# Theta's tiles in three parts around the second attention's transposes and values, v ahead of q and k, and the sines of three tiles in a row

## What is computed

```python
# 1: masked attention over 8 heads of 64 channels (4 local, 4 strided)
attn = softmax(where(mask[h], 0.125 * q @ k.T, -1e9)) @ v         # x: (4, 576, 512)
# 2: mixing over tokens and channels
theta = x @ w_theta
y = w_tok_r @ (x * cos(theta)) + w_tok_i @ (x * sin(theta))
u = x + y
x2 = u + maximum(u @ w_ch, 0)
# 3: four causal attention experts, two of which count for each token
gate = softmax over the 2 largest of (x2 @ w_gate)
out = sum_e gate[e] * softmax(causal(0.125 * (x2 @ wq[e]) @ (x2 @ wk[e]).T)) @ (x2 @ wv[e]) @ wo[e]
```

## Times and profile before

| | us |
|---|---|
| median of 3 runs (630.7 to 634.88) | 632.44 |
| the profiled execution, whole | 630.41 |
| its span in the trace | 628.6 |
| PE busy | 561.1 (89%) |
| DVE busy | 355.3 (57%) |
| ACT busy | 260.8 (41%) |
| POOL busy | 125.1 (20%) |
| granted TensorE clock, mean | 0.973 of full |

### The profile page before, as it was taken

The page is one execution under the profiler, slowest core; times in us unless marked ns, Lnnn a source line. Parts: engine busy times, 40 slices in busy tenths (PEclk is TensorE's granted clock), DMA queues, the critical chain, the costliest instruction groups (busy, mean ns, idle before and its releaser), DMA issues.

```text
span 628.6 us, 11634 instructions
## 1 busy us (share of the span) xinstructions
PE 561.1 (89%) x4469; PEld 474.6 (75%) x4469; DVE 355.3 (57%) x835; ACT 260.8 (41%) x768; POOL 125.1 (20%) x128
## 2 busy tenths in 40 slices
PE   6776999999988989999988989999988889999777
PEld 4555679998865679998865679998856669998545
DVE  1466384666778641566778641575776832344462
ACT  1556263365442362365442362255533353112343
POOL 2012162001321142001321133001221215000110
PEclk9878999999999999999999989999989999999989
DMA  6900315321000012321000012330000010000002
GB/s 158 276 22 19 101 34 124 89 58 26 14 2 1 18 59 59 90 54 26 14 1 2 18 59 50 83 69 22 18 2 1 5 70 3 1 2 1 1 0 76
DMA packets 73413, 27.13 MB, mean 43 GB/s; under 512 B 68624, under 2 KB 68624, under 8 KB 73360
## 3 DMA queue, kind: packets, MB, share of 16 engines
q1 hardware_dynamic: 70992, 22.70, 14.5%
q10 hardware_dynamic: 2368, 3.70, 1.7%
HBM read 21.67 MB, written 4.72 MB: 42 GB/s over the span
## 4 chain that ended last, share of the span: by engine, by line
PE 72%; DVE 14%; ACT 6%; issue 4%; POOL 1%; ACTq 1%; DVEq 0%; POOLq 0%
PE acc L1126 34%; PE wide L1126 14%; PE wide L1210 4%; PE turned L1286 4%; PE wide L1189 3%; PE turned L1243 3%; PE turned L1230 3%; DVE xt L961 2%; PE turned L1152 2%; PE acc L1396 2%; ACT probs L757 2%; PE turned L1260 2%; PE wide L1174 1%; DVE probs L935 1%; DVE turns L983 1%
## 5 line engine op out<-in xcount | busy, mean ns | idle before, releaser
L689 POOL TENSOR_TENSOR probs<-probs,rec 96x768 f32<-96x768 f32 (+1 forms) x16 | 21.7, 1355 | 231.5 <-DVE rec L919 231.5
L764 ACT ACTIVATE probs<-wide,nmax 128x128 f32<-128x128 f32 (+4 forms) x72 | 39.1, 549 | 67.3 <-DVE nmax L904 64.9
L757 ACT ACTIVATE probs<-wide,nmax 96x128 f32<-96x128 f32 (+1 forms) x176 | 61.5, 370 | 10.3 <-issue 6.7
L772 ACT ACTIVATE pt<-turned 128x384 f32<-128x384 f32 (+3 forms) x64 | 30.9, 483 | 83.3 <-PE turned L1230 43.7
L698 POOL TENSOR_TENSOR probs<-probs,weight 128x128 f32<-128x128 f32 (+4 forms) x36 | 27.0, 769 | 167.4 <-DVE weight L942 167.4
L1126 PE MATMUL wide<-w_tok_hi,z_hi 128*128 128x288 f32 x216 | 46.8, 297 | 2.7 <-ACT o_sb L790 1.3
L948 DVE COPY pt<-turned 128x288 f32<-128x288 f32 (+4 forms) x72 | 32.0, 454 | 27.2 <-PE turned L1243 25.2
L1126 PE MATMUL wide<-w_tok_lo,z_hi 128*128 128x288 f32 x216 | 45.8, 293 | 0.0
L1126 PE MATMUL wide<-w_tok_hi,z_lo 128*128 128x288 f32 x216 | 45.8, 293 | 0.0
L711 POOL TENSOR_TENSOR z_lo<-absf,z_hi 128x512 fp32r<-128x512 f32 x20 | 28.3, 1415 | 70.2 <-ACT z_hi L820 70.2
L904 DVE TENSOR_REDUCE nmax<-wide 128x1 f32<-128x128 f32 (+4 forms) x72 | 32.7, 510 | 16.1 <-PE wide L1215 16.1
(11 more groups left out here) (170 smaller groups left out, 1491.2 us busy)
## 6 DMA issues: line engine op xcount, KB each, us to landing
raw_q<-in_q SPq DMA_DIRECT2D x32, 128.0 KB, 2.4
raw_k<-in_k SPq DMA_DIRECT2D x32, 128.0 KB, 2.4
out<-o_sb SPq DMA_DIRECT2D x16, 256.0 KB, 2.0
raw_v<-in_v SPq DMA_DIRECT2D x64, 31.5 KB
raw_v<-in_v SPq DMA_DIRECT2D x16, 120.0 KB
raw_r<-in_moe_w_tok_r ACTq DMA_DIRECT2D x1, 1152.0 KB, 9.0
stage<-in_moe_w_theta ACTq DMA_DIRECT2D x2, 512.0 KB, 5.5
raw_i<-in_moe_w_tok_i ACTq DMA_DIRECT2D x1, 1024.0 KB, 10.9
```

The source lines that it names most:

```text
L689: g.tensor_tensor(pr, pr, rec[0:rows, 1, 0:nt].unsqueeze(2).broadcast_to([rows, nt, w]), ALU.mult).then_inc(s["probs_pool"], 1)
L757: e = a.activation(probs[0:rows, hh, t * P:t * P + w], wide[slot][0:rows, t * P:t * P + w], ACT.Exp, bias=nmax[0:rows, hh, t:t + 1], accum ...
L764: e = a.activation(probs[:, hh, to0:to0 + n], wide[slot][:, at0:at0 + n], ACT.Exp, bias=nmax[:, hh, j:j + 1], accum_out=sums[:, hh, j:j + 1])
L772: ins = a.activation(dst, src, ACT.Copy)
```

## The change

It edits the lists of the bodies, and what a body's steps need for it:

- `theta` of tiles 0 to 3 becomes three steps on the contraction's four chunks: chunks 0 and 1 where the whole was (before turn 1), chunk 2 after turn 1, chunk 3 after the values. All three add into one place of `acc`, and the eviction stays at the slot's end. `slot_of_s3` no longer evicts at once between its steps.
- In the slots of stage 1 `v` comes ahead of `qk`: four v in slot 1; v 4, two qk and `rank` in slot 2; three qk in slot 3 and three in slot 4. Before: four qk; four v; v 4, `rank` and two qk; two qk. A slot's number is its place in FILL, from 0.
- `trig` 0, 1 and 2 stand together at the end of the slot with theta 3, ahead of `out` 0. `products` 0 goes ahead of the last unit's transposes, `products` 1 ahead of its values, and theta 4 is evicted ahead of `products` 1 (before: after the values).
- `last_slot` gives the order of the last unit's slot; in the epilogue it puts out 2, 3 and 4 behind the values (before, out 2 and 3 stood around turn 1).
- The first wave waits for its four PSUM places one by one, where it first writes each, rather than for all at its start.

```diff
@@ slot_of_s3
-    steps += gap[0] + [("turn",) + behind + (1,)]
-    if ahead:
-        steps += [("norm",) + ahead + (0,), ("exp",) + ahead + (1,)]
-    steps += at_once(gap[1]) + [("values",) + behind]
-    if ahead:
-        steps.append(("norm",) + ahead + (1,))
-    return steps + done(gap[0]) + at_once(gap[2]) + at_once(gap[3])
+    steps += gap[0] + [("turn",) + behind + (1,), ("norm",) + ahead + (0,), ("exp",) + ahead + (1,)]
+    steps += gap[1] + [("values",) + behind] + gap[2] + [("norm",) + ahead + (1,)]
+    return steps + done(gap[0] + gap[1] + gap[2]) + at_once(gap[3])
+def last_slot(behind, gap):
+    steps = gap[0] + [("turn",) + behind + (0,)] + gap[1] + [("turn",) + behind + (1,)] + gap[2]
+    return steps + [("values",) + behind] + gap[3]
...
+def theta_in_parts(m):
+    return [[("theta", m, 0, 2)], [("theta", m, 2, 3)], [("theta", m, 3, KC)]]
@@ FILL
-    [halves("qk", 0)[:1], halves("qk", 0)[1:], halves("qk", 2)[:1], halves("qk", 2)[1:]],
     [v_of(0), v_of(1), v_of(2), v_of(3)],
-    [v_of(4), [("rank",)], [("gexp",)] + halves("qk", 1)[:1], [("gate",)] + halves("qk", 1)[1:]],
-    [halves("qk", 3)[:1], halves("qk", 3)[1:]],
-    [theta(0)],
-    [theta(1)],
-    [theta(2)],
-    [theta(3), [], out_of(0)],
-    [theta(4), [("trig", 0), ("products", 0)] + out_of(1),
-     [("trig", 1), ("products", 1), ("split", 0)] + out_of(2, 3, 4)],
+    [v_of(4), halves("qk", 0)[:1], halves("qk", 0)[1:], [("rank",)]],
+    [halves("qk", 2)[:1], [("gexp",)] + halves("qk", 2)[1:], halves("qk", 1)[:1], [("gate",)]],
+    [halves("qk", 1)[1:], halves("qk", 3)[:1], halves("qk", 3)[1:]],
+    theta_in_parts(0),
+    theta_in_parts(1),
+    theta_in_parts(2),
+    theta_in_parts(3) + [[("trig", 0), ("trig", 1), ("trig", 2)] + out_of(0)],
+    [[("products", 0)], theta(4), at_once(out_of(1)) + [("done", "theta", 4), ("products", 1)],
+     [("split", 0)] + at_once(out_of(2, 3, 4))],
@@ FILL_LAST
-    [out_of(2), out_of(3), out_of(4)],
+    [[], [], [], at_once(out_of(2, 3, 4))],
@@ PE, wave
-                        for n in range(4):
-                            free(("wide", "acc")[n // 2], n)
...
+                            if m == 0 and n == 0:
+                                for i in ((0,), (1,), (2, 3))[o]:
+                                    free(("wide", "acc")[i // 2], i)
```

More of the change, by code:

```diff
@@ L61, with result @@
 EVICTED = ("channel", "qk", "v", "theta", "out")
+def result(step):
+    return step[:2] if step[0] == "theta" else step
 def done(steps):
-    return [("done",) + x for x in steps if x[0] in EVICTED]
+    return [("done",) + result(x) for x in steps if x[0] in EVICTED and x[3:] in ((), (KC,))]
 def at_once(steps):
@@ L86, in attention_steps @@
         if behind and behind[0] == "s3":
-            steps += slot_of_s3(ahead, behind, gap)
+            steps += slot_of_s3(ahead, behind, gap) if ahead else last_slot(behind, gap)
             continue
@@ L122, in slot_of_s3 @@
 def slot_of_s3(ahead, behind, gap):
-    steps = [("turn",) + behind + (0,)]
-    if ahead:
-        steps += [("scores",) + ahead, ("max",) + ahead + (0,), ("max",) + ahead + (1,), ("exp",) + ahead + (0,)]
-    steps += gap[0] + [("turn",) + behind + (1,)]
-    if ahead:
-        steps += [("norm",) + ahead + (0,), ("exp",) + ahead + (1,)]
-    steps += at_once(gap[1]) + [("values",) + behind]
-    if ahead:
-        steps.append(("norm",) + ahead + (1,))
-    return steps + done(gap[0]) + at_once(gap[2]) + at_once(gap[3])
+    steps = [("turn",) + behind + (0,), ("scores",) + ahead, ("max",) + ahead + (0,), ("max",) + ahead + (1,),
+             ("exp",) + ahead + (0,)]
+    steps += gap[0] + [("turn",) + behind + (1,), ("norm",) + ahead + (0,), ("exp",) + ahead + (1,)]
[4 more added lines that the diff above has]
+    return steps + [("values",) + behind] + gap[3]
 def halves(kind, *os):
@@ L230, in psum_uses @@
         return ["wide"] * 2
+    if k == "theta":
+        return ["acc"] if step[2:3] in ((), (0,)) else []
     if k == "wave":
         return ["wide"] * 2 + ["acc"] * 2 if step[1] == 0 else []
-    return {"out": ["acc"], "theta": ["acc"], "products": ["turned"], "mix": ["wide"], "channel": ["acc"],
+    return {"out": ["acc"], "products": ["turned"], "mix": ["wide"], "channel": ["acc"],
             "qk": ["acc"], "v": ["acc"], "wtok": ["acc"] * 2, "tail": ["turned"]}.get(k, [])
@@ L1312, in emit @@
                         pe.wait_ge(s["xl"], c.at("xl"))
-                    slot = free("acc", 0)
-                    for kc in range(KC):
+                    kc0, kc1 = step[2:4] or (0, KC)
+                    if kc0 == 0:
+                        note[("theta", m)] = free("acc", 0)
+                    slot = note[("theta", m)]
+                    for kc in range(kc0, kc1):
                         ins = split_matmuls([(acc[slot][0:rows, :], None)], [x[:, kc, t0:t0 + rows] for x in xu],
                                             [lambda _, x=x, kc=kc: x[:, kc, :] for x in w_th], kc == 0, kc == KC - 1)
-                    ins.then_inc(full["acc"][slot], 1)
+                    if kc1 == KC:
+                        ins.then_inc(full["acc"][slot], 1)
                 elif kind == "products":
```

11 lines of the change are left out of this document (7 added, 4 removed).

## The result

| | before | changed |
|---|---|---|
| median of five runs, us | 632.84 (630.70 to 634.88) | 613.29 (608.12 to 615.51) |
| the profiled execution, whole | 630.41 | 608.12 |
| its span | 628.6 | 606.3 |
| PE, DVE busy in it | 561.1, 355.3 | 552.3, 360.1 |
| its mean granted clock | 0.973 | 0.986 |

The ratio is 0.969, with a 95% interval of 0.965 to 0.973: the change makes the kernel 19.5 us faster. I had forecast 10.8 us (621.6). The direction holds and the time lies inside the range, 612.5 to 628.5, but near its lower end: nearly half of the gain is not in my sum. That the range holds, by 0.8 us, is partly luck: I had set that end for one rival coming true at a time, and what came was a term of wrong size with a rival in part. In a second comparison of five rounds (the last experiment) the ratio is 0.971, 0.967 to 0.974.

The account below looks back on a forecast made before the run. PE, a queue of matmuls with holes, was taken as the bound. Terms of 2.2 + 1.2 + 0.3 = 3.7 us a body, 11.1 in three, less 0.3 for the epilogue, gave 10.8 us: 621.6 us, range 612.5 to 628.5.

Parts of the forecast that it names:

- term 1: Slots of stage 3: theta in parts covers PE's waits ahead of the values and for `at_lo`; 2.2 us a body.
- term 2: Out 0 to first wave: the last slot's new order removes 2.6 us of waits, adds 1.4; gain 1.2 us a body.
- term 3: Seam of stages 1 and 3: v sooner shrinks 2.9 us of waits, stretched `rank` adds 2.3; gain 0.3 us a body.
- epilogue: Out 2 and 3 no longer cover POOL's work and copies behind turn 1, `at_lo`'s wait is covered; +0.3 us, once.
- The first rival: Stage 1, slot 2: POOL doesn't hold `rank` up, or PE doesn't wait; 2.1 us a body more, 615.3; chance 0.20.
- the clock falls less: In the bodies, closed holes keep PE's clock up; 5.1 us at stake, 616.5 us; chance 0.10.
- In other stretches than before: Condition for being wrong: PE's clock falls in other stretches of the body than in the kernel before; no size given.
- the parts only move the wait: Slots of stage 3: DVE and ACT set the pace, theta's parts gain 0; 628.2 us; chance 0.17.
- The clock falls more: Behind the new waits of 2.3 and 1.4 us PE's clock drops, each body loses 5 us; 636.6 us; chance 0.05.

Follow-up runs that it names:

- the last experiment: The changed kernel itself, unedited, timed again beside the kernel before: 612.37 us, ratio 0.971 to the kernel before.
- experiment 1: Changed kernel with theta's three parts put back into one step ahead of turn 1: 627.75 us, ratio 0.992 to the kernel before.
- experiment 7: Changed kernel with the first wave waiting at its start for all four places at once: 614.93 us, a single profiled execution.
- experiment 9: Kernel before with theta in parts as its only edit in the bodies (epilogue and `slot_of_s3` list as changed): 622.72 us, ratio 0.987 to the kernel before.
- experiment 4: Changed kernel with the last unit's slot and the sines ordered as before; parts, seam and single waits kept: 615.67 us, ratio 0.974 to the kernel before.
- experiment 6: Changed kernel with theta in two parts, chunks 0 and 1 before turn 1, 2 and 3 after it, none behind the values: 622.08 us, once.
- experiment 5: Changed kernel with only `trig` 0 ahead of out 0, `trig` 1 and 2 back where they were: 615.68 us, a single profiled execution.
- experiment 3: Changed kernel with `rank` moved one group earlier in slot 2, ahead of the second half of qk: 603.48 us, ratio 0.956 to the kernel before.
- experiment 2: Changed kernel with the old order of qk, v and `rank` in slots 1 to 4 of stage 1: 614.81 us, ratio 0.973 to the kernel before.
- experiment 8: Changed kernel with `rank` ahead of the second half of qk and out 1 behind products 0: 599.73 us, ratio 0.947 to the kernel before.

## Why the prediction was right, and what it missed

| us | forecast | measured |
|---|---|---|
| term 1, a body (B) | 2.2 | 2.22 |
| term 2, a body (C) | 1.2 | 2.09 |
| term 3, a body (A) | 0.3 | 0.63 |
| three bodies | 11.1 | 14.8 |
| epilogue | -0.3 | -0.64 |
| clock | 0 | about 5, in another comparison 3; 3.1 in the bodies of the traces |
| sum | 10.8 | 19.5 |

**Term 1** holds in size and in how it comes about. The waits ahead of the values are 1.1 us where I named 1.2, that for `at_lo` is gone, and experiment 1 brings them back with the theta step alone. In B, PE's idle time fell by 2.5 us (32.00 - 28.18 to 29.80 - 28.49) while its busy time rose by 0.3. By the timeline a new start costs 0.08 to 0.11 us (0.31 to 0.34 to the next matmul where 0.23 is the usual distance), so the eight cost about 0.8 as priced; that busy time rose by less goes with the ends of matmuls that no longer stand alone (see term 2).

**Term 2** is the step that was mis-sized. The mechanism was right: the removed waits are gone, and the one it adds is 1.38 us where I had 1.4. What failed is "2.6 us by the stretch", where I took PE's length minus its busy time for what the holes cost. The same 106 instructions at full clock are busy for 15.02 us before and 14.17 after. The 0.85 us of difference are the ends of matmuls that overlap the next one when there is one, and stand alone ahead of a hole (experiment 7). So C's four holes cost 2.6 + 0.85 = 3.5 us against a C with one hole; 3.5 - 1.4 = 2.1, as measured. The Trainium skill ("Perfetto Trace Analysis", Identifying the Most-Contended Engine) says that matmul busy time is a poor measure of how near PE is to its limit, because matmuls are pipelined; these rows agree, with two busy times for the same matmuls. By experiments 9, 7 and 4 the 2.09 us split into three: 0.73 from theta's parts, 0.68 from the wave's single waits, 0.69 from the new order of the last slot. I had credited none of it to the parts. They matter here because theta 3's last three matmuls cover DVE's work behind the values: in the old order what went was the wait of 0.35 us ahead of theta 4 (0.60 by the starts; 0.11 more is out 0's start, which moved into B), and in the new one it is 0.68 us of the wait for products 0 (experiment 6). The sines cost nothing, as said (experiment 5).

**Term 3** went as told. `rank` took 3.75 us where I had 4, two of its operations over 1 us, and PE waited 2.0 us where I had 2.3. The wait for the first probabilities fell to 0.3. The smaller new wait is the 0.3 us by which the term was short. The first rival, rank not held up, priced 2.1 us a body; experiment 3 took the stretch away, and `rank` out of the copy's way with it, and got 2.2.

**Epilogue.** From out 0 to the end it took 15.54 us and now takes 16.18, both at full clock. I had given up 1.1 for the cover of turn 1 and taken 0.8 back; PE now waits 1.1 us for copies (0.6 and 0.5) that had been covered, and the 0.8 is gone.

**Clock.** The rival "the clock falls less" had 5.1 us at stake and a chance of 0.10, and it came true in part, beside the forecast rather than in its place: the bodies of before lost 4.6 us to the clock and those of the changed kernel 1.5, in one trace of before and two of the changed kernel. The two stretches of the earlier trace rows have no counterpart in the changed kernel's bodies; one fall of 1.5 us is left in A of the first. I treated as rivals two things that go together: the holes behind which the clock fell, theta 4's eviction (1.3 us) and the seam (1.8), are among those that the terms close, and the fall that is left follows the hole that term 3 adds. "In other stretches than before" was a condition on which I would be wrong, and it partly holds (A of the first body, in both traces), without deciding anything.

Of the other rivals, "the parts only move the wait" fell with B (29.8, not 32.0 us). "The clock falls more" did not happen in the changed kernel, but does in experiments 1 and 6, where the hole ahead of theta 4 is 2.06 instead of 1.38 us (1.6 us lost in C and 1.5 in A of each body of experiment 6, where the rival needed 3.6).

## What to carry to other kernels

Price a hole on PE from the starts of the matmuls around it, against the distance of the same pair where nothing waits, and not from length minus busy time: a hole gave 0.2 us more than its listed wait where I compared starts (0.25 ahead of theta 4, 0.24 ahead of the wave). In B the parts' new starts took more than that away: the waits fell by 2.8 us and the stage by 2.2. Look at what a step follows on its own engine and whom that releases: seven small DVE operations cost 2 us more because they stood right behind the reciprocal that starts POOL, and moving them by one step, which also took them out of the way of a copy, was worth 2.2 us a body, where the whole change was worth 4.9. And split a long product so that its last part covers the eviction of what the next step needs, not only the wait in its own slot.

## What was not expected of the hardware

A DVE operation with a single small input of SBUF is held up by POOL too. In slot 3 of the changed kernel:

```profile
304.60 0.18 DVE L1112 TENSOR_TENSOR gate<-gate,grec 128x20 f32<-128x20 f32 x1
304.81 1.27 DVE L1113 COPY gate_last<-gate 64x2 f32<-64x2 f32 x1
306.10 0.16 DVE L1114 COPY gate_last<-gate 64x2 f32<-64x2 f32 x1
```

The copy of 64 x 2 numbers takes 1.27 us and its twin 0.16, and it ends 0.02 us after POOL's operation of 304.66, which runs for 1.40 us. The Trainium skill ("SBUF — State Buffer", Who interferes with whom) lists copy and tensor_scalar among those that can take the shared ports in a 2-port mode; by that rule the row is as it should be, and so is the 1.11 us of line 1091, but I had counted only operations with two inputs.

In the bodies of the twelve traces every fall of PE's clock to half starts within 2 us of the end of a hole of 1.3 to 2.1 us, lasts some 3.5 us (7 in one case) and costs about 1.5 us (or 3). Whether a hole is followed by one depends on its place as much as on its length:

| the hole, and the kernels that have it | us | bodies with a fall behind it |
|---|---|---|
| products 0: experiments 1, 6 | 2.05 to 2.07 | 6 of 6 |
| the copy behind `rank`: changed (twice), experiments 1, 4, 5, 6, 7 | 1.97 to 1.99 | 11 of 21 |
| the seam: before, experiments 2, 9 | 1.81 to 1.85 | 4 of 9 |
| products 0: changed (twice), experiments 2, 3, 5, 7 | 1.36 to 1.38 | 0 of 18 |
| theta 4's eviction: before, experiments 4, 9 | 1.30 to 1.32 | 1 of 9 |

From the first body to the end of C of the third, experiments 3 and 8, which have none of the holes over 1.4 us, kept the full clock. No run shows why one body has the fall and the next, with the same hole, has not.
